# A convolution-and-mixing kernel: x loaded in pieces of 16, 112 and 128 rows, and a new order of work

## The reference

```
w    = softmax(weight)                       # 8 heads x 7 taps
y    = conv(x, w)                            # per head, over this row and the 6 before
wq   = y @ w_q;  wk = y @ w_k                # 192 -> 64
W    = (wq @ wk.T) / 8                       # 4224 x 4224 in each batch
out  = relu(W @ y) @ w_out                   # 192 -> 192, float32
```

## Time and profile before

| | |
|---|---|
| median of 3 runs | 173.91 us (172.88 to 174.39) |
| the profiled execution | 174.98 us, its span 173.2 us |
| PE busy | 159.3 us, 92% of the span |
| DVE, ACT busy | 127.1 us (73%), 118.5 us (68%) |
| mean granted clock of TensorE | 0.977 of full speed |
| moved by DMA | 40.67 MB, 235 GB/s on average |

### The profile page before, as it was taken

How to read it: one execution, slowest core, us unless ns; L and a number is a source line. 1 busy time by engine, 2 the same in 40 slices (tenths; PEclk the granted TensorE clock), 3 DMA queues, 4 the chain that set the end, 5 groups by cost and what they waited for, 6 DMA issues and landing times.

```text
span 173.2 us, 6345 instructions
## 1 busy us (share of the span) xinstructions
PE 159.3 (92%) x2824; PEld 119.7 (69%) x2827; DVE 127.1 (73%) x222; ACT 118.5 (68%) x229; POOL 28.8 (17%) x37
## 2 busy tenths in 40 slices
PE   5799999999999999999899999999859999999950
PEld 1368958777587786778767976699738777886630
DVE  4484797978778799957678798964752798666970
ACT  3232678789955899677677699978343898679800
POOL 7999252523430000000000000000000000000000
PEclk9999999999999999999999999999996999999995
DMA  4999999999999999999999894129950467588796
GB/s 111 206 190 188 205 191 193 192 195 189 193 191 289 341 218 192 282 340 326 340 225 186 226 392 165 49 99 388 388 225 4 182 261 298 222 309 316 289 364 231
DMA packets 47991, 40.67 MB, mean 235 GB/s; under 512 B 36451, under 2 KB 40797, under 8 KB 47965
## 3 DMA queue, kind: packets, MB, share of 16 engines
q0 software_dynamic: 35072, 13.21, 63.7%
q1 hardware_dynamic: 11536, 25.69, 40.8%
q10 hardware_dynamic: 1356, 1.37, 2.4%
HBM read 27.53 MB, written 25.95 MB: 309 GB/s over the span
## 4 chain that ended last, share of the span: by engine, by line
PE 72%; DMA 12%; DVE 6%; issue 3%; ACT 2%; SPq 1%; ACTq 1%; DVEq 0%
PE ps L344 17%; PE ps L861 13%; PE ps L338 13%; DMA out_dram<-out_sb 9%; PE ps L337 6%; PE ps L348 5%; PE ps L744 4%; PE ps L773 4%; DMA out_sb<-in_x_dram 3%; PE ps L339 3%; PE ps L975 3%; PE ps L783 2%; DVE out_sb L1063 2%; PE ps L349 2%; ACT out_sb L1063 2%
## 5 line engine op out<-in xcount | busy, mean ns | idle before, releaser
L683 ACT CAST y<-ps 122x432 bf16<-122x432 f32 (+4 forms) x59 | 35.4, 649 | 17.6 <-PE ps L339 10.9
L991 ACT ACTIVATE rt<-ps 128x512 bf16<-128x512 f32 (+3 forms) x52 | 31.7, 647 | 10.1 <-PE ps L344 8.1
L1063 ACT COPY out_sb<-ps 128x768 f32<-128x768 f32 (+2 forms) x43 | 30.4, 724 | 7.0 <-PE ps L344 4.2
L861 PE MATMUL ps<-y 122*64 122x64 bf16 (+6 forms) x816 | 34.1, 224 | 0.1
L683 DVE CAST y<-ps 122x432 bf16<-122x432 f32 (+4 forms) x38 | 25.3, 689 | 10.8 <-PE ps L339 6.5
L861 PEld LDWEIGHTS ps<-y 122*64 122x64 bf16 (+2 forms) x816 | 30.6, 112 | 3.8 <-issue 0.8
L1063 DVE COPY out_sb<-ps 128x768 f32<-128x768 f32 (+2 forms) x35 | 27.3, 799 | 6.7 <-PE ps L339 3.2
L566 POOL DMA_DIRECT2D xw<-in_x_dram x32 | 28.3, 899 | 23.0 <-issue 7.6
L992 DVE TENSOR_SCALAR rt<-ps 128x512 bf16<-128x512 f32 (+2 forms) x36 | 26.8, 766 | 3.0 <-PE ps L344 1.9
L714 DVE COPY ytl<-ps 128x976 bf16<-128x976 bf16 (+1 forms) x40 | 22.8, 590 | 3.3 <-PE ps L348 1.9
L344 PE MATMUL ps<-woh,rt 64*128 64x192 bf16 (+1 forms) x238 | 21.3, 250 | 0.3 <-DVE out_sb L1063 0.2
(11 more groups left out here) (137 smaller groups left out, 247.0 us busy)
## 6 DMA issues: line engine op xcount, KB each, us to landing
out_dram<-out_sb SPq DMA_DIRECT2D x28, 768.0 KB, 7.2
xw<-in_x_dram POOLq DMA_DIRECT2D x7, 816.0 KB, 31.2
xw<-in_x_dram POOLq DMA_DIRECT2D x7, 768.0 KB, 29.2
out_dram<-out_sb SPq DMA_DIRECT2D x6, 384.0 KB, 4.3
xw<-in_x_dram POOLq DMA_DIRECT2D x2, 432.0 KB, 9.2
out_dram<-out_sb ACTq DMA_DIRECT2D x2, 384.0 KB, 4.5
out_dram<-out_sb SPq DMA_DIRECT2D x3, 192.0 KB, 3.9
out_sb<-in_x_dram SPq DMA_DIRECT2D x2, 192.0 KB, 4.4
```

The costliest lines, as they stand in the source:

```text
L683: return e.copy(dst, src) if op.engine == "ACT" else e.tensor_copy(dst, src)
L861: mm = e.matmul(bank(where.bank)[p : p + n, o : o + z - a], Y[0:w, yb, c, r : r + n], Y[0:w, yb, c, a:z], start=begin and o == 0, stop=end ...
L991: return e.activation(dst, src(), AF.Relu)
L1063: return e.copy(dst, src) if op.engine == "ACT" else e.tensor_copy(dst, src)
```

## The change

Three things. **Loads.** Of the first eight chunks, ACT now issues rows 16 to 127 of chunks 0 to 3 in one transfer; SP issues, behind the weight, rows 0 to 15 of chunks 1 to 3, rows 6 to 15 of chunk 0, and then chunks 4 to 7 whole; each of the four has a semaphore of its own, and the casts wait for all transfers of their group. On GpSimd the first chunk of a batch is two transfers, 112 rows and 10. The last chunk is read with 128 rows in one transfer with the chunks ahead of it, running into the next batch (what it holds beyond row 82 feeds no row of y that is used); only the last batch, where nothing follows, has 80 rows and 2 apart. **The zeroing** of the last chunk's rows is gone. **The order.** `PLAN` is a new table, so the place of nearly every operation, many forms of matmuls, and the engine of many copies differ. Lines move by two or three: L525 is now L527, L537 is L539, L1071 is L1074.

```diff
...
-PLAN = """1D 38A 2D 8D 47G 39A 0S 4D 40A 5D 21A 6D 14G 3D 22D 48G 23D 15D 24A 20D 25D 26D 49G 16F6 17C7 18F1 27D 43S 28F5 29F2 19A 30D 31C4 44S 50G 42D 33A 41D 32A 34C3
...
+PLAN = """0S 37A 38S 1D 45G 2D 4D 5D 20A 13G 6D 3D 21D 22D 14D 39S 15F7 23A 19D 24D 25D 26D 16C2 17F6 27F1 29D 41D 42S 49S 48S 18A 28F2 46G 30C5 33C4 32A 31A 34D 40D 35D
...
@@ -379,7 +379,6 @@
     zero_x0 = [
         add("DVE", lambda e, op: e.memset(XW[0 : KC - 1, 1:, 0, :], 0.0), 700, vt=0),
     ]
-    zero_x = add("DVE", lambda e, op: e.memset(XW[64:128, :, NCC - 1, :], 0.0), 800, vt=-8.7)
     zero_q = add("DVE", lambda e, op: e.memset(WQH[:, :, :], 0.0), 130, vt=-8.6)
     zero_k = [
         add("DVE", lambda e, op: e.memset(WKT[64:128, :, :], 0.0), 100, vt=-8.55),
@@ -492,7 +491,7 @@
             bands.append(add("ACT" if half == 0 else "DVE", band, 320, drains=fill))
     run_3 = run_up(1, after=fills)
 
-    turns = [zero_r, one, zero_x, eps, zero_t, zero_f, zero_s, mx, sub, step, own, sm, rc, wn, taps, *bands[2:]]
+    turns = [zero_r, one, eps, zero_t, zero_f, zero_s, mx, sub, step, own, sm, rc, wn, taps, *bands[2:]]
     turns += [zero_q, *zero_k, zero_m, zero_o, zero_x0[0]]
     for p, op in zip(turns, turns[1:]):
         op.after.append(p)
@@ -502,43 +501,48 @@
     x_read = {}
     at = [5000.0]
     last_load = []
-    s_xf = [semaphore(f"s_xf{i}") for i in range(2)]
+    head = [load_w]
+
+    HEAD = (
+        (("ACT", 0, 16, 128, 0, 4), ("SP", 1, 0, 16, 1, 4), ("SP", 2, KC - 1, 16, 0, 1)),
+        (("SP", 3, 0, 128, 4, 8),),
+    )
 
     def gen_load(b, gi):
         sem = semaphore(f"s_x{b}_{gi}")
         cs = groups_of(b)[gi]
         parts = []
         base = b * S * D
-        full = [c for c in cs if 0 < c < NCC - 1]
+        full = [c for c in cs if 0 < c < NCC - (b == B - 1)]
         if cs[0] == 0 and b > 0:
-            parts.append((XW[KC - 1 : 128, b % NX, 0, :], bass.AP(x_t, base, [[D, CW], [1, D]])))
+            for p, z in ((16, 128), (KC - 1, 16)):
+                parts.append((XW[p:z, b % NX, 0, :], bass.AP(x_t, base + (p - KC + 1) * D, [[D, z - p], [1, D]])))
         if b == 0 and gi < 2:
             assert cs == list(range(4 * gi, 4 * gi + 4)) and NXF == 8
-            load[b, gi] = []
-            before = [load_w] if gi else []
-            for k, steps in enumerate((((4, 6), (6, 8)) if gi else ((0, 1), (1, 2), (2, 4)))):
-
-                def emit(e, op, steps=steps):
-                    c0, cz = steps
-                    p = KC - 1 if c0 == 0 else 0
-                    src = bass.AP(x_t, base + (CW * c0 - KC + 1 + p) * D, [[D, 128 - p], [CW * D, cz - c0], [1, D]])
-                    return e.dma_start(XF[p:128, c0:cz, :], src)
-
-                got = add(
-                    "SP" if gi else "ACT", emit, 900, after=before, dma=(f"xf{gi}", s_xf[gi], 16), tail=2800, vt=-9.8 if gi == 0 else -8.9)
-                got.descs = 128 * (steps[1] - steps[0])
-                before = [got]
-            if gi == 0:
-                early.after.append(got)
-            for c0, cz in ((4 * gi, 4 * gi + 2), (4 * gi + 2, 4 * gi + 4)):
-                load[b, gi].append(
-                    add(
-                        both,
-                        lambda e, op, c0=c0, cz=cz: (e.copy if op.engine == "ACT" else e.tensor_copy)(
-                            XW[:, 0, c0:cz, :], XF[:, c0:cz, :]
-                        ),
-                        {"ACT": 56 + (cz - c0) * D / 0.99, "DVE": 62 + (cz - c0) * D / 1.5},
-                        needs=[got, *([zero_f] if c0 == 0 else [])], after=bands if gi else [ex, taps], vt=-7.4 + gi, kind="narrow"))
+            got = []
+            for engine, k, p, z, c0, cz in HEAD[gi]:
+
+                def emit(e, op, p=p, z=z, c0=c0, cz=cz):
+                    src = bass.AP(x_t, base + (CW * c0 - KC + 1 + p) * D, [[D, z - p], [CW * D, cz - c0], [1, D]])
+                    return e.dma_start(XF[p:z, c0:cz, :], src)
+
+                got.append(
+                    add(engine, emit, 900, after=head[-1:] if engine == "SP" else [], dma=(f"xf{k}", semaphore(f"s_xf{k}"), 16), tail=2800, vt=-9.8 + k * 0.1))
+                got[-1].descs = (z - p) * (cz - c0)
+                if engine == "SP":
+                    head.append(got[-1])
+                else:
+                    early.after.append(got[-1])
+            load[b, gi] = [
+                add(
+                    both,
+                    lambda e, op, c0=c0, cz=cz: (e.copy if op.engine == "ACT" else e.tensor_copy)(
+                        XW[:, 0, c0:cz, :], XF[:, c0:cz, :]
+                    ),
+                    {"ACT": 56 + (cz - c0) * D / 0.99, "DVE": 62 + (cz - c0) * D / 1.5},
+                    needs=[*got, *([zero_f] if c0 == 0 else [])], after=bands if gi else [ex, taps], vt=-7.4 + gi, kind="narrow")
+                for c0, cz in ((4 * gi, 4 * gi + 2), (4 * gi + 2, 4 * gi + 4))
+            ]
             at[0] += 1000
             return
         n = len(full)
@@ -548,14 +552,13 @@
                 bass.AP(x_t, base + (CW * full[0] - KC + 1) * D, [[D, 128], [CW * D, n], [1, D]]),
             )
         )
-        if cs[-1] == NCC - 1:
-            rows = S - (CW * (NCC - 1) - KC + 1)
-            parts.append(
-                (
-                    XW[0:rows, b % NX, NCC - 1, :],
-                    bass.AP(x_t, base + (CW * (NCC - 1) - KC + 1) * D, [[D, rows], [1, D]]),
+        if b == B - 1 and cs[-1] == NCC - 1:
+            first_row = CW * (NCC - 1) - KC + 1
+            rows = S - first_row
+            for p, z in ((0, rows - rows % 16), (rows - rows % 16, rows)):
+                parts.append(
+                    (XW[p:z, b % NX, NCC - 1, :], bass.AP(x_t, base + (first_row + p) * D, [[D, z - p], [1, D]]))
                 )
-            )
 
         at[0] += len(cs) * 260.0
         load[b, gi] = []
@@ -565,7 +568,7 @@
                 "POOL",
                 lambda e, op, part=part: e.dma_start(*part),
                 900,
-                needs=[*{id(r): r for c in cs for r in x_read.get((b - NX, c), [])}.values(), *([zero_x] if cs[-1] == NCC - 1 else [])],
+                needs=[*{id(r): r for c in cs for r in x_read.get((b - NX, c), [])}.values()],
                 after=[*last_load, *([] if first else [ident])],
                 dma=(f"x{b}_{gi}", sem, 16),
                 vt=-10 if first else -4 + b + gi * 0.1 + 0.02 * k,
@@ -667,7 +670,7 @@
 
             ev_needs = [r for r in y_read.get((b - NY, "all"), [])]
             mm = add(
-                "PE", conv, mm_ns(n * GRP, 2), needs=[*load[b, gi], bands[hp], *([zero_x] if cs[-1] == NCC - 1 else []), *([zero_x0[0]] if b and c0 == 0 else [])], after=[*ev_needs, run_3, *conv_first], drains=run_3 if (b, gi, hp) == (0, 0, 0) else None, banks=nb, vt=vt, whole=True, kind="conv")
+                "PE", conv, mm_ns(n * GRP, 2), needs=[*load[b, gi], bands[hp], *([zero_x0[0]] if b and c0 == 0 else [])], after=[*ev_needs, run_3, *conv_first], drains=run_3 if (b, gi, hp) == (0, 0, 0) else None, banks=nb, vt=vt, whole=True, kind="conv")
             for c in cs:
                 x_read.setdefault((b, c), []).append(mm)
             conv_first[:] = conv_first or [mm]
```

## The result

The changed kernel takes 168.58 us (median of 4 runs, 168.23 to 169.61) against 173.74 (4 runs, 172.88 to 174.39) for the kernel before: a ratio of 0.9716, 95% interval 0.9655 to 0.9776. It is faster by about 2.8%. Timed again later, beside the last experiments, it took 169.29 (6 runs, 167.84 to 170.52) against 173.39, a ratio of 0.9801 (0.9737 to 0.9864). The forecast was 169.3, within 167.5 to 173.1.

A forecast was written before the change was run, and what follows sets the result against it. PE was taken to bound the kernel, with its start and two stops. From 174.98 us, 0.9 (start), 2.64 (stops) and 1.7 (slow clock) gave 169.7; set against the median, 169.3 was taken, own range 167.5 to 171.0, whole range to 173.1.

The forecast's parts named there:

- The stops: PE's two unexplained waits, before 122.71 and 129.87 us: late instruction blocks under a store burst; the new order saves 2.64 us.
- The first two rivals: PE's two stops remain or move (0.15), or are no instruction fetch and no order moves them (0.05); both 173.0 us.
- rival (1): PE's two stops remain or move to another place in the new order; only the start gains, 173.0 us; chance 0.15.
- The slow clock behind them: PE's lower 1.2 GHz level from 131.0 to 134.5 us, after the second stop, goes with the stops: 1.7 us saved.
- The start: Up to PE's first convolution: x lands earlier through new load row counts; 0.9 us saved, bounds 0 and 1.1.
- the taps' end: DVE's work ahead of the first cast of x at the start, taken to end at 5.76 us.
- the ninth chunk as a floor: GpSimd's load of the ninth chunk is not surely faster, so PE can pull ahead there by 0.94 us at most.
- The third rival: The start gains nothing, since x lands by bytes or the ninth chunk holds PE: 170.2 us; chance 0.12.
- The fourth rival: Six large stores together delay a copy into its output slot, last landing after 22 us; slower, up to 178 us; chance 0.07.
- The work of PE: PE's matmul time under the new order and forms: change taken as 0, bounds -0.8 and +0.5 us.

The follow-up runs named there:

- loads_only: The changed kernel's new loads with the old order of the kernel before: 170.87 us, ratio 0.9874 to the kernel before.
- chunk0_split: The kernel before with only chunk 0's 122 rows cut into 112 and 10, both issued by ACT: 173.94 us, ratio 1.0081 to before.
- before_fewer: The kernel before with 22 products near the stops written at full width instead of two halves, 158 instructions fewer: 171.30 us, ratio 0.9829 to before.
- order_only: The kernel before with the new order but the old loads: 170.62 us, ratio 0.9781 to the kernel before.
- after_g106: The changed kernel with GpSimd's two transfers of a batch's first chunk cut as 106 and 16 rows, not 112 and 10: 169.45 us, ratio 0.9803 to before.
- after_denser: The changed kernel with 26 products from 96 to 128 us written as halves again, 208 instructions more: 171.25 us, ratio 0.9798 to before.
- after_again: The changed kernel unaltered, timed again beside the last experiments: 169.29 us, ratio 0.9801 to the kernel before.
- after_122: The changed kernel with ACT's first transfer taking 122 rows of each of four chunks instead of 112: 181.41 us, ratio 1.0468 to before.
- after_best: The changed kernel with both DVE casts of x ahead of the bands and chunks 4 to 7 loaded by ACT behind its first transfer: 167.45 us, ratio 0.9727.
- before_light_stores: The kernel before with SP's six stores of 114.92 to 121.85 us writing only 192 of 768 columns: 169.64 us, ratio 0.9785 to before.

## Why the prediction was right, and where it was wrong

**The stops: right, in cause and size.** The forecast took both as late blocks and dropped 2.64 us. They are gone with the new order alone, with fewer instructions alone, and with lighter stores alone, and stayed with the new loads alone. That what came late was a block of instructions is inferred, from the counts between and before the stops; no row shows a block on its way. The first two rivals fall with that; rival (1) has a point left, since a denser stretch brought 0.40 us back at another place. The page of the Trainium skill that I had set against it, "Runtime: NRT & Kernel Launch", section "Instruction fetch mechanics", says that crossing a block is mostly hidden. In this kernel it is for all but two of 22 packets; at those two a burst of stores met two dense blocks in a row, and they cost 0.85 and 1.79 us.

**The slow clock behind them: right for this profile, too large for the median.** 1.7 us was taken out as a part of every run. Remainders show it in the profile: 150.5 - 146.2 = 4.3 = 2.64 + 1.7. But loads_only and chunk0_split had the two stops (2.8 and 2.3 us) and no dip behind them, and their remainders are 150.0 (0.6 of it the wait for x) and 148.1. In the 11 runs of the kernel before in the last group, the mean clock was 0.977, as in its profile, in two (174.72 and 175.13 us); the other nine have 0.985 to 0.993 and 171.7 to 174.3 us. The profile that I worked from was among the slowest executions of its kernel. So the term that failed is the 1.7 us, as a part of every run: the median lay 1.07 below 174.98, which the forecast put down to shorter stops, and this clock can account for it.

**The start: the transfers' gain right, the event wrong.** The forecast was 0.9. The first convolution (7.43) and the ninth chunk (8.63) came earlier than forecast (7.6 to 8.3, near 10.0), and the profiles differ by 2.4 at the copy into `gsb`. At the full clock, the loads' part alone is 20.40 (before_fewer) - 19.25 (loads_only) = 1.15, or 20.26 (order_only) - 18.99 to 19.30 (after_g106, after_denser) = 1.0 to 1.3. The rest of the 2.4, 1.1 to 1.4, is the clock: before's profile lost 22.71 - 20.40 = 2.3 by it, after's 20.29 - 19.1 = 1.2 or so. So 0.9 was a little small, for two reasons that the prediction had wrong. It took the taps' end as fixed at 5.76; they came 0.9 earlier. The weight, 8 rows that SP issues at the same 0.80, landed at 2.17 and not 3.48, and ACT, with one issue for three, began its table load at 1.23 and not 2.27; in chunk0_split, where only the weight was early, the taps stayed at 5.46. And it took the ninth chunk as a floor near 10, since GpSimd's queue is not touched; SP's first weight load, which waits for that chunk, stands at 8.51, and at 8.96 in loads_only. That the other transfers are out of its way sooner is a guess that no run tests. Against these stands the second cast of 1.09 us, which held the first convolution at 7.43; in after_again the same cast took 0.35 and the convolution stood at 6.55, with a wait of 1.41 behind it for SP's load. That the total came so near the median is in part luck, since the two errors, a start that gained a little more and a clock that most runs had not lost, had opposite signs: 4.6 us less than the median of the kernel before was forecast, and 5.2 and 4.1 were measured.

**The third rival** (bytes alone) falls with after_122. But the row count that the forecast set against it is not enough by itself, as chunk0_split shows. Its other half, the ninth chunk as the floor, holds further on: in after_best nothing else is left ahead of it.

**The fourth rival**: the six full stores did come together, but cost PE nothing. SP sent them behind a small one, seven in all, from 62.85 to 67.78 us, and the last landed after 18.7 us where 22 was forecast (15.2 in the kernel before). One copy waited for one of them, on ACT:

```profile
77.57 1.50 ACT L1066 COPY out_sb<-ps 128x768 f32<-128x768 f32 x2 [0.57 <-DMA out_dram<-out_sb]
```

PE waited for none of it; the wait of 0.2 us in its list stands at 62.49, ahead of the burst. No copy waited for the last stores, so the copies that need their slots stand further on, as the prediction's point against this rival had it.

**The work of PE: right.** Taken as 0 within -0.8 and +0.5. Remainders without stops are 146.0 for the old order (before_light_stores) and 146.2 to 146.6 for the new. One reading in it was wrong: a product of full width is not always as cheap as a pair of halves, as the 147.2 of before_fewer shows.

## What to carry to other kernels

An idle stretch of the bounding engine without a releaser is worth a count of instructions to the next one: if it is one fetched block, both the density of the code there and what loads the DMA engines at that time are to be looked at, and taking away either was enough here. A load from a plain queue with a row count like 122 is worth cutting into 112 and 10, but the cut alone may bring nothing: here it paid with a single early issue on ACT, and lost 0.8% where it added an issue there. And a single profile can hold a slow clock that most runs don't have: before its loss is put into a sum against the median, a second profile of the same kernel or the clocks of its runs should show it too.

## What the runs showed that I had not expected

A transfer of 366 KB with 122 rows took 18.4 us, and one of 336 KB with 112 rows 3.0 us; I had expected x at 9 us or later and a time of 175 at most. The slow transfer also held up the weight's 224 bytes on another queue (4.74 instead of 2.17 us).

TensorE's clock at the start is not set by the kernel alone: with the same work it stood on the lower level (1.2 GHz) for 3.4 us (4.2 x 0.41 x 2, from 0.59 over 4.2 us) in two profiles and not at all in others, and over a part of the start the clock's column says 1.00 while the matmuls step by 0.18 us instead of 0.09.

A dense stretch of 4 us with 213 instructions under a full burst of stores passes without a stop when sparse ones stand around it.
